# A recurrence, a gated MLP and a mixer on one core: the diagonal as one number per token and head, scores one chunk ahead, and the deviations worked out for two tiles at a time on GpSimd

## The reference

```python
for t in range(S):                               # attention, per batch and head
    y[t] = r[t] @ (state + outer(u * k[t], v[t]))
    state = w[t][:, None] * state + outer(k[t], v[t])
x = y, heads side by side                        # (B, 768, 384)
h = gelu_tanh(x @ w_in)                          # (B, 768, 1024), u and v its halves
v_n = (v - mean(v)) / sqrt(var(v) + 1e-6) * g_ln
x = x + (u * (w_sg @ v_n + b_sg[:, None])) @ w_out
x = x + (relu(x.T @ tok1) @ tok2).T              # tok 256
x = x + relu(x @ ch1) @ ch2                      # ch 1536
```

## Time and profile before

| what | value |
| --- | --- |
| runs | 384.88, 386.17, 390.32 us; median 386.17 us |
| profiled execution | 387.06 us |
| its span | 385.6 us |
| mean granted clock of TensorE | 0.987 |
| busy: TensorE, VectorE, ScalarE, GpSimd | 364.2, 163.2, 105.9, 176.3 us |
| transfers of v, `vn<-in_v_both` | 12 of 416 KB, 9.6 us from issue to landing |

### The profile page before, as it was taken

The page is one execution under the profiler, slowest core; times in us unless marked ns, Lnnn a source line. Parts: engine busy times, 40 slices in busy tenths (PEclk is TensorE's granted clock), DMA queues, the critical chain, the costliest instruction groups (busy, mean ns, idle before and its releaser), DMA issues.

```text
span 385.6 us, 7208 instructions
## 1 busy us (share of the span) xinstructions
PE 364.2 (94%) x2926; PEld 323.6 (84%) x2926; DVE 163.2 (42%) x293; ACT 105.9 (27%) x197; POOL 176.3 (46%) x181
## 2 busy tenths in 40 slices
PE   6875889999599999999999999999999999999996
PEld 5754778899599989999999999888888888888885
DVE  7997469885044414123432677331013310133110
ACT  4566425565140018340000334320012300033000
POOL 6776499999539998635999930000000000000000
PEclk9999899999799999999999999999999999999999
DMA  8999639821202020030214300000100001000001
GB/s 226 288 310 276 194 111 243 242 92 43 83 2 82 2 81 2 3 82 2 82 43 125 122 2 2 0 0 3 53 27 2 0 0 56 27 0 2 0 30 53
DMA packets 13954, 28.82 MB, mean 75 GB/s; under 512 B 1888, under 2 KB 6496, under 8 KB 13920
## 3 DMA queue, kind: packets, MB, share of 16 engines
q1 hardware_dynamic: 13920, 28.34, 25.3%
HBM read 25.98 MB, written 2.36 MB: 73 GB/s over the span
## 4 chain that ended last, share of the span: by engine, by line
PE 84%; issue 1%; ACT 1%; DVE 1%; DVEq 0%; ACTq 0%
PE bank L1109 77%; PE bank L1188 3%; PE bank L1205 1%; PE bank L1129 1%; PE bank L1239 1%; PE bank L1139 1%; PE bank L1151 1%; ACT uT L779 0%; ACT sg_hi L835 0%; ACT win_hi L835 0%; DVE bank L962 0%; ACT xT_hi L816 0%; DVE xr L962 0%; DVE xr L1043 0%; DVE st L954 0%
## 5 line engine op out<-in xcount | busy, mean ns | idle before, releaser
L790 ACT ACTIVATE ha_hi<-bank 128x512 fp32r<-128x512 f32 x36 | 21.5, 598 | 100.5 <-PE bank L1109 100.5
L1035 DVE SCALAR_TENSOR_TENSOR ha_lo<-bank,ha_hi 128x512 fp32r<-128x512 f32 x36 | 24.9, 692 | 49.7 <-ACT ha_hi L790 49.7
L1109 PE MATMUL bank<-u2T_hi,c_hi 128*128 128x512 f32 x108 | 42.1, 389 | 0.0
L1109 PE MATMUL bank<-u2T_lo,c_hi 128*128 128x512 f32 x108 | 42.0, 389 | 0.0
L1109 PE MATMUL bank<-ha_hi,c_lo 128*128 128x512 f32 x108 | 42.0, 389 | 0.0
L1109 PE MATMUL bank<-ha_lo,c_hi 128*128 128x512 f32 x108 | 42.0, 389 | 0.0
L1109 PE MATMUL bank<-ha_hi,c_hi 128*128 128x512 f32 x108 | 42.0, 389 | 0.0
L1109 PE MATMUL bank<-u2T_hi,c_lo 128*128 128x512 f32 x108 | 42.0, 389 | 0.0
L1109 PE MATMUL bank<-sg_hi,z_lo 128*128 128x384 f32 x96 | 33.5, 349 | 4.1 <-issue 4.1
L1109 PE MATMUL bank<-sg_hi,z_hi 128*128 128x384 f32 x96 | 33.2, 346 | 0.0
L1109 PE MATMUL bank<-sg_lo,z_hi 128*128 128x384 f32 x96 | 33.2, 346 | 0.0
(11 more groups left out here) (136 smaller groups left out, 838.0 us busy)
## 6 DMA issues: line engine op xcount, KB each, us to landing
krT<-in_kr_turned SPq DMA_DIRECT2D x12, 448.0 KB, 8.7
vn<-in_v_both SPq DMA_DIRECT2D x12, 416.0 KB, 9.6
raw<-in_moe_w_ch SPq DMA_DIRECT2D x12, 384.0 KB, 3.1
raw<-in_moe_w_sg SPq DMA_DIRECT2D x6, 384.0 KB, 4.6
out<-xr SPq DMA_DIRECT2D x8, 256.0 KB, 2.0
raw<-in_moe_w_in SPq DMA_DIRECT2D x4, 384.0 KB, 12.4
raw<-in_moe_w_tok SPq DMA_DIRECT2D x4, 384.0 KB, 3.5
wz<-in_w_turned SPq DMA_DIRECT2D x6, 225.8 KB, 7.9
```

The source lines that it names most:

```text
L790: sc.activation(ha[0][:, i, :], bank[:, :], ACT.Relu).then_inc(act_out, 1)
L1035: ve.scalar_tensor_tensor(ha[1][:, i, :], bank[:, :], 0.0, ha[0][:, i, :].bitcast(F32), ALU.max, ALU.subtract).then_inc(dve_out, 1)
L1109: ins = te.matmul(dst, left[l], right[r], start=first and l == 1, stop=last and (l, r) == (0, 0))
```

## The change

- The diagonal becomes one number per token and head: four products with `rk` as weights and two columns of u moving, `dg_cols`, 8 numbers per token. VectorE multiplies v by them into `vd` (two buffers). The outputs begin with three products that add `vd`, turned over by the identity, to all 128 rows of the bank `by`; so `y_tile` and the turned copy of v go (the tile of v shrinks from 832 to 512 words a partition). In chunks 0 to 4 ScalarE copies the result (`take_y`), from chunk 5 on `x_tile` reads the bank itself.
- TensorE's order: state products of n, scores, turned keys and diagonal of n + 1, then the outputs of n. `am` and, in the first chunks, the score banks have two buffers. From chunk 5 on the outputs come before the state products, and then the diagonal of n + 1.
- ScalarE takes `kn(n+1)` in turn n; the first `rp` is made by GpSimd.
- `SLOT` is filled anew: v(0,0) goes from chunk 5 to chunk 6, and sg(0,0) out of chunk 11 into `TAIL`. GpSimd makes scale(6) before the lo part of w_in 2, and that of w_in 3 in chunk 5. The sg pieces are made one a chunk, two in chunk 10.
- `rstd_pair` does two tiles with the same three instructions; VectorE writes the negated mean.
- 14 narrow and 22 full products run ahead of the first scores in place of 54 narrow ones.

```diff
 SLOT = {
-    5: [("u", 0, 0), ("u", 0, 2), ("v", 0, 0)],
-    6: [("v", 0, 1), ("v", 0, 2)],
...
-    11: [("u", 0, 7), ("sg", 0, 0)],
+    5: [("u", 0, 0), ("u", 0, 2)],
+    6: [("v", 0, 0), ("v", 0, 1)],
...
+    11: [("u", 0, 5), ("u", 0, 7)],
 }
...
-            def rstd_tile(b, tc):
-                n = NC * b + tc
-                pool.wait_ge(stat, n + 1)
-                gp.tensor_scalar(rstd[:, tc:tc + 1], mv[:, tc, 1:2], 1e-6, None, ALU.add).then_inc(rstd_a, 1)
...
+            def rstd_pair(b, tc):
+                at_ = slice(tc, tc + 2)
+                half = (NC * b + tc) // 2
+                pool.wait_ge(negated, NC * b + tc + 2)
+                gp.tensor_scalar(rstd[:, at_], mv[:, at_, 1], 1e-6, None, ALU.add).then_inc(rstd_a, 1)
+                pool.wait_ge(rstd_a, half + 1)
+                gp.tensor_tensor(rstd[:, at_], rstd[:, at_], nhalf[:, :], ALU.pow).then_inc(rstd_done, 1)
+                pool.wait_ge(rstd_done, half + 1)
+                gp.tensor_tensor(shift[:, at_], nmean[:, at_], rstd[:, at_], ALU.mult).then_inc(shifted, 1)
...
+            def take_y(n):
+                act.wait_ge(av_done, n + 1)
+                sc.copy(x_cols(n), tiles(by)).then_inc(y_done, 1)
...
+            take_k(0)
             for n in range(YR):
-                take_k(n)
                 if n:
+                    take_y(n - 1)
                     take_state(n - 1)
+                if (n + 1) % NC < NC - 1:
+                    take_k(n + 1)
                 for i in checks[n]:
                     check_range(i)
                 if n > 1:
                     xt_high(n - 2)
...
-                ve.tensor_tensor(t1[:, :], dg_bank(n)[:, 0:C], vn[:, n % VR, VW:VW + C], ALU.mult).then_inc(t1_done, 1)
+                ve.tensor_tensor(vd[:, n % 2, :].rearrange("s (p i d) -> s p i d", p=NP, i=2),
+                                 dg_cols(n).rearrange("s (p i a) -> s p i a", p=NP, a=1).to_broadcast([PART, NP, 2, D]),
+                                 vn[:, n % VR, :].rearrange("s (p i x) -> s p i x", p=NP, i=2)[:, :, :, 0:D], ALU.mult).then_inc(vd_done, 1)
...
+                pe.wait_ge(vd_done, n + 1)
+                for a in range(KC):
+                    te.matmul(by[:, tile(a)], vd[:, n % 2, tile(a)], ident[:, :], start=a == 0, stop=False)
...
-                for a in range(KC):
-                    for g in range(4):
-                        p, j = divmod(4 * a + g, 3)
-                        ins = te.matmul(dg_bank(n)[32 * g:32 * g + 32, tile(a)], ubd[0:QP, p, 32 * j:32 * j + 32],
-                                        rk[0:QP, n % 2, p, :], start=True, stop=True)
-                        yield
+                for p in range(NP):
+                    ins = te.matmul(dg_cols(n)[:, 2 * p:2 * p + 2], rk[0:QP, n % 2, p, :], ubd[0:QP, p, :], start=True, stop=True)
                 ins.then_inc(dg_done, 1)
...
+            scores(0)
+            turn_kp(0)
+            diagonal(0)
             for n in range(YR):
-                scores(n)
-                turn_kp(n)
-                rest_of(diagonal(n))
                 rest_of(state_products(n))
+                scores(n + 1)
+                if (n + 1) % NC < NC - 1:
+                    turn_kp(n + 1)
+                diagonal(n + 1)
                 if n == YR - 1:
                     sum_range()
                 rest_of(outputs(n))
```

More of the change, by code:

```diff
@@ L48 @@
 RAW = H * PJ * D
+DCOL = NP * D
 W_LOW, W_HIGH = 0.72, 1.38
@@ L699, in rest @@
                     split_piece("ch2", i)
-            scale_k(0)
+            scale(0)
             rk_products(0)
@@ L955, in state @@
                                  ).then_inc(st_done, 1)
-            def y_tile(n):
-                dve.wait_ge(av_done, n + 1)
-                dve.wait_ge(t1_done, n + 1)
-                src = tiles(y_bank(n))
-                ve.tensor_tensor(x_cols(n) if n < YR else src, src, tiles(t1), ALU.add).then_inc(y_done, 1)
             def x_tile(n):
@@ L1077, in _ @@
                 mask(n, 1)
-                if n == YR:
-                    y_tile(n - 1)
                 if n + 2 < NCH:
@@ L1084, in _ @@
                     stats(b, i)
-                diagonal(n)
-                y_tile(n)
                 x_tile(n)
+                if n + 1 < NCH:
+                    diagonal(n + 1)
                 if n % NC < NC - 1:
                     state(n)
-            take_job("sg", 0, 0)
             for t, (kind, b, i) in enumerate(TAIL):
@@ L1179, in parts @@
                             new.append((v0 + 16, 2 * p + 1))
-                        here = old + [(vn[:, n % VR, c:c + 32], am[:, h, :]) for c, h in new]
-                        todo += [(a, left, right, e == 0, e == len(here) - 1) for e, (left, right) in enumerate(here)]
+                        here = old + [(vn[:, n % VR, c:c + 32], am[:, n % 2, h, :]) for c, h in new]
+                        todo += [(a, left, right, a == KC - 1 and e == len(here) - 1) for e, (left, right) in enumerate(here)]
                     return todo
@@ L1186, in outputs @@
                         if part:
-                            a, left, right, first, last = part
-                            ins = te.matmul(yb[32 * g:32 * g + 32, tile(a)], left, right, start=first, stop=last)
+                            a, left, right, last = part
+                            ins = te.matmul(by[32 * g:32 * g + 32, tile(a)], left, right, start=False, stop=last)
                             yield
@@ L1292, in product, with keep_busy @@
                 ins.then_inc(mm_done, 1)
-            def keep_busy(m):
-                for i in range(m):
+            def keep_busy(narrow, full):
+                for i in range(narrow):
                     te.matmul(ps[6][32 * (i % 4):32 * (i % 4) + 32, 0:PART], ident[:, 0:32], ident[:, :], start=True, stop=True)
+                for i in range(full):
+                    te.matmul(ps[6][:, 0:PART], ident[:, :], ident[:, :], start=True, stop=True)
             pe.wait_ge(ident_made, 1)
@@ L1314, in _ @@
             for n in range(YR, NCH):
-                scores(n)
-                if n % NC < NC - 1:
-                    turn_kp(n)
+                if n > YR:
+                    scores(n)
+                    if n % NC < NC - 1:
+                        turn_kp(n)
                 for job in round_jobs(n):
                     product(*job)
-                rest_of(diagonal(n))
                 rest_of(outputs(n))
```

155 lines of the change are left out of this document (73 added, 82 removed).

## The result

The changed kernel takes 388.31 us as a median of 20 runs (386.92 to 390.11), the kernel before beside it 386.69 us (383.78 to 391.70, 20 runs). The ratio is 1.0049 with an interval of 1.0027 to 1.0070: half a per cent slower, where 1.4% faster was forecast. The profiled span grew from 385.6 to 386.7 us.

The account below looks back on a forecast made before the run. The start of sg(0,1) on TensorE settles the gain: v(0,0) at 52.5 us plus 51.8 us gives 104.3 against 109.78 us, 5.5 us sooner, so 381.6 us profiled and 380.7 us median; range 377.3 us less 1.5 us to 386.3 us.

Parts of the forecast that it names:

- the ring of the first chunks: First chunks: rp(n+1), scores, turned keys, kn, ScalarE's checks and cast, then GpSimd's xT_lo, kp, rp(n+2); rp(5) ends at 38.6 us.
- What starts the ring: First chunks: masks of chunk 2 come about 0.9 us sooner than 21.23 us, and kn(3) starts at about 22.9 us.
- The turn of the ring: First chunks, n = 2 and 3: one turn takes 8.7 us, including 3.2 us for ScalarE's checks and cast.
- GpSimd to `v(0,0)`: GpSimd's queue after rp(5), with 0.9 us for loading verdict and flag: 13.85 us, so v(0,0) can start at 52.5 us.
- TensorE from `v(0,0)` to `sg(0,1)`: TensorE's v and u pairs, chunks 6 to 11 and sg(0,0) at full clock: 51.8 us, so sg(0,1) starts at 104.3 us.
- A rule against the state products: Diagonal's weight loads: 0.7 us for eight at the state products' rate; the skill's rule gives 0.85 us, 0.8 us more over five groups.
- The stop before `sg(0,0)`: TensorE's stop at 97 us and the slow clock behind it, 4.1 + 2.9 = 7.0 us, would be gone.
- The spare: Before sg(0,0): GpSimd's last sg_lo needs 6.0 us after chunk 10's outputs, TensorE 7.8 us, leaving 1.8 us.
- Rival B: sg(0,0) still waits: 1.2 us of stop and 2.9 us of slow clock remain, 384.8 us; chance 0.10.
- Rival A: TensorE's new diagonal work is at the cheap end, zero instead of +0.57 us on six chunks: 377.3 us; chance 0.20.
- Rival C: Slower: TensorE holes, as if instructions came late, fall into both ring turns, moving v(0,0) by 6.3 us: 387.0 us; chance 0.08.
- Rival D: GpSimd's pairs cost two tiles each, so it is 2.2 us ahead instead of 5.8: 380.7 us; forecast with it 0.62.

Follow-up runs that it names:

- run 7: run 2's kernel with the hi part of the first w_in piece made one turn of ScalarE sooner; 383.02 us, ratio 0.9901.
- run 10: Changed kernel with 11 instead of 22 full products in the warm-up and nothing else; 386.20 us, ratio 1.0006.
- run 1: Changed kernel with the warm-up back to 54 narrow products and no full ones; 387.77 us, ratio 1.0016.
- run 2: Changed kernel with ScalarE's cast xT_hi(n-2) moved to the head of its turn, ahead of kn(n+1) and the range checks; 382.20 us, ratio 0.9881.
- Run 4: Changed kernel with one diagonal product instead of four in chunks 7 to 11, leaving out part of the term, for time only; 385.12 us.
- run 3: Changed kernel with both the 54 narrow warm-up products and ScalarE's cast first in its turn; 383.25 us, ratio 0.9894.
- run 8: run 7's kernel with 11 instead of 22 full products in the warm-up; 380.15 us, ratio 0.9824.
- run 5: Changed kernel with the deviations worked out one tile at a time again, the rstd pairs undone; 388.73 us, ratio 1.0056.
- run 9: run 8's kernel with the last range check, the sum over the checks and the count placed sooner; 383.23 us in six runs, ratio 0.9812.

## Why the prediction was wrong

**The step that failed is the start of `v(0,0)`**: forecast at 52.5 us, found at 56.62 us. The prediction had the ring of the first chunks start too early, because it gave the new warm-up no term. A second term was too small: TensorE's work from `v(0,0)` on, by 2.5 us. The order of events in that later part it read correctly.

- *What starts the ring.* `kn(3)` was forecast at 22.9 us and came at 26.71 us. The warm-up had no term in the sum, and no reason was given for that. The change has 22 products of full width in it, listed as a part of the change, and their 44 records take 7.26 us (6.27 us in the profile of run 7), where the kernel before had only narrow ones and the first `rp` was the later of the two. It holds the first scores until 10.85 us, 2.6 us after the first `rp` is there; run 10 gets 2.9 us of `rp(4)` back by halving it. The rest, 0.9 us, is mostly TensorE's: in run 10 the masks of chunk 2 come at 20.48 us, as the estimate of VectorE's gain has it (21.23 - 0.9), but `kn(3)` only at 23.81 us, since TensorE needs 3.3 us for what was allowed 2.6 us. That the transfers of v come in time held for the changed kernel. Where the first chunks start sooner it does not: VectorE waits 1.14 us for one in run 1 and 1.40 us in run 10.
- *The turn of the ring.* Forecast 8.7 us, found 42.52 - 33.63 = 8.9 us. The mechanism, checks and cast of ScalarE in front of `kp` and `rp`, is right, and run 2 shows its price: 3.4 us a turn. But the ring stops TensorE for 3 us, and behind that stop the clock is at its lower level: the diagonal and the identity products of chunk 4 take 3.3 us instead of 1.9. The prediction had read how the clock falls behind the stop at 97 us, and did not ask it of the stop that the new ring makes. In the kernel after it moved `rp(5)` little, since ScalarE's checks and cast stand in the ring and wait only for `kn`. In runs 1 and 10 it reaches the scores too, and their turns last 10.2 and 9.7 us; it takes back 1.3 of 1.8 us and 0.8 of 2.9 us that the shorter warm-up gives.
- *GpSimd to `v(0,0)`.* Forecast 13.85 us, found 56.62 - 42.52 = 14.1 us: right in sum, but by luck. The verdict was given 0.9 us and cost 0.1 us, and a wait of 0.82 us for a cast, which was not forecast, took its place.
- *TensorE from `v(0,0)` to `sg(0,1)`.* Forecast 51.8 us, found 54.3 us. The diagonal was sized too low: 0.98 us instead of 0.7 us for eight records, five of them 1.4 us. The three identity products are right, 0.67 against 0.66 us. The outputs take 1.68 instead of 1.58 us (0.5 us in five) and 0.13 us more in chunk 6, the first v pair 0.2 and the last u pair 0.16 us more. Run 4 shows the price of a record. That it goes by the 128 columns of weights, and not by the two that move, is read from the old diagonal beside it: 32 columns of weights, 128 moving, 0.033 us a record.
- *A rule against the state products.* The Trainium skill ("TensorE: Matmul & The Clock Gate", LDWEIGHTS) lets a load take its columns over 1.2, in ns, an estimate of 107 ns here, and the prediction set the rate of the state products against it. Run 4 measured 0.112 us a record and the chain 0.12 us: the rule was the nearer of the two, and following it would have closed about 0.8 of the 2.5 us.
- *The stop before `sg(0,0)`* is gone, with its slow clock: right, 7.0 us. The spare was forecast at 1.8 us and is 1.2 us (last `sg_lo` until 106.59, `sg(0,0)` at 107.76). Rival B did not come.
- *Rival A* (cheap TensorE work) fell with the diagonal. *Rival C* (slower) had the right sign and the wrong mechanism: the 2.99 us in front of scores(4) end with `rp(4)`, 33.63 us, so they are the ring itself and no instructions that come late. Holes of the other sort do exist in the ring (1.58 us inside the diagonal of chunk 4 in run 3, where it cost 0.9 us) and off it (run 8). *Rival D* (pairs do not save): they do, 1.26 us for a pair against 1.2 us for a single tile, and run 5 shows that the time is the same either way.

Sum: 4.1 us late at `v(0,0)` and 2.5 us in TensorE's work make 6.6 us, and with the 5.5 us that were forecast as gain this is the 1.1 us by which the span grew. Of the 4.1 us the shorter warm-up gives back 2.3 us in run 10; of the other 1.8 us, 0.9 us lie in the start of the ring and 1.0 us in its turn, which the half clock makes longer there.

What stays open: why the clock falls behind some holes and not behind others. In run 8 it stays at 1.00 behind a hole of 2.74 us; in run 7 it is at 0.57 behind one of 0.59 us; in run 9 the same program has executions of both sorts. No run here separates what decides it.

## What to carry to other kernels

When a change lets one engine's result feed the next turn of a ring, list what each engine has queued ahead of the instruction in the ring, and put long work that nobody waits for (here range checks) behind what the ring needs; that one line was worth 5.9 us. Price every part of a diff against the time at which its engine would otherwise start, the warm-up too: it is free only up to that time (11 products, not 22). And before a job's resources are rebuilt, try to put other work into its stop: one job moved in the old kernel gained about as much (0.9866) as the repaired change did in run 2 (0.9881).

## What the hardware showed that was not expected

- A matmul with 128 columns of weights is not cheap for moving only two columns: 0.11 to 0.12 us a record on the path at full clock, against 0.033 us for the 24 records of the old diagonal, which moved 128 columns over 32 columns of weights.
- Full products in a warm-up may buy clock, but that is not shown: with 22 or 11 of them the granted clock from 10 to 20 us was 1.00 in every profile, without them it was 0.66 in run 3 and 1.00 in run 1 and in the kernel before.
- One program can run at two mean clocks. Run 9's six executions differ by 7.4 us in span, three at 0.999 to 1.0 and three at 0.986 to 0.987. What sets off one or the other is open.
- The power on GpSimd costs 0.57 us for one column and 0.72 us for two.
